# Attention turns the next heads before the probabilities, and the two feed-forward blocks are reordered at their group borders

## The reference

```python
# attention: q, k, v are (2, 8, 768, 64); proj is (64, 6)
q_bucket = sum over 6 bits of (q @ proj > 0) * 2**bit;  k_bucket likewise
scores = where(q_bucket == k_bucket, q @ k.T / 8, -1e9)
attn = exp(scores - max);  attn = attn / (sum + 1e-9);  out = attn @ v
x = out, heads side by side, (1536, 512)
# first feed-forward block, 512 -> 1536 -> 512
x = (sigmoid(x @ w_gate) * (x @ w_val)) @ w_out
# second feed-forward block, 512 -> 2048 -> 512
h = x @ w_in
g = where(h >= 1, h, where(h <= -1, 0, (h + 1)**2 / 4))
out = g @ w_out2
```

## Time and profile before

| | |
|---|---|
| median of 3 runs | 798.59 us (798.53 to 802.11) |
| profiled execution | 800.75 us, its span 799.0 us |
| granted TensorE clock, mean | 0.998 |
| PE busy | 778.3 us (97%) |
| PEld busy | 718.2 us (90%) |
| DVE busy | 564.7 us (71%) |
| ACT busy | 457.1 us (57%) |
| POOL busy | 551.4 us (69%) |

### The profile page before, as it was taken

The page is one execution under the profiler, slowest core; times in us unless marked ns, Lnnn a source line. Parts: engine busy times, 40 slices in busy tenths (PEclk is TensorE's granted clock), DMA queues, the critical chain, the costliest instruction groups (busy, mean ns, idle before and its releaser), DMA issues.

```text
span 799.0 us, 12190 instructions
## 1 busy us (share of the span) xinstructions
PE 778.3 (97%) x4403; PEld 718.2 (90%) x4403; DVE 564.7 (71%) x867; ACT 457.1 (57%) x731; POOL 551.4 (69%) x533
## 2 busy tenths in 40 slices
PE   7999999999999999999999999999999999999998
PEld 6899999998979999999899999988999988899996
DVE  5888888887888576446975655597678677666554
ACT  4888988988997424335434334454455464534543
POOL 4667767778889998877885887776657756466420
PEclk9999999999999999999999999999999999999999
DMA  7896586475100212202021221111121111101002
GB/s 146 183 191 138 134 174 139 82 153 119 54 1 27 77 58 79 77 29 79 27 80 54 80 80 53 53 54 54 37 71 53 47 32 69 65 26 53 1 1 79
DMA packets 61930, 60.08 MB, mean 75 GB/s; under 512 B 28384, under 2 KB 51632, under 8 KB 61872
## 3 DMA queue, kind: packets, MB, share of 16 engines
q1 hardware_dynamic: 61712, 59.32, 28.8%
q10 hardware_dynamic: 160, 0.00, 0.0%
HBM read 37.75 MB, written 3.15 MB: 51 GB/s over the span
## 4 chain that ended last, share of the span: by engine, by line
PE 77%; DVE 8%; ACT 6%; issue 5%; POOL 3%; DMA 0%; SPq 0%; POOLq 0%; DVEq 0%; ACTq 0%
PE ps L748 11%; PE ps L749 11%; PE ps L750 11%; PE ps L778 8%; PE ps L789 5%; PE ps L791 5%; PE ps L790 5%; PE ps L779 4%; PE ps L714 4%; ACT ph L907 2%; PE ps L731 2%; PE ps L732 2%; PE ps L702 2%; DVE probs L1200 2%; PE ps L705 2%
## 5 line engine op out<-in xcount | busy, mean ns | idle before, releaser
L748 PE MATMUL ps<-xop,wset 128*128 128x384 f32 x560 | 191.2, 341 | 5.0 <-DVE u L1276 3.9
L749 PE MATMUL ps<-xop,wset 128*128 128x384 f32 x560 | 189.5, 338 | 0.0
L750 PE MATMUL ps<-xop,wset 128*128 128x384 f32 x560 | 189.0, 338 | 0.0
L1276 DVE TENSOR_TENSOR u<-ps,u 128x384 f32<-128x384 f32 x144 | 79.5, 552 | 102.0 <-PE ps L750 101.8
L516 POOL TENSOR_TENSOR wset<-stage,wset 128x512 fp32r<-128x512 f32 x39 | 54.3, 1392 | 122.0 <-ACT wset L955 122.0
L748 PEld LDWEIGHTS ps<-xop,wset 128*128 128x128 f32 x560 | 105.4, 188 | 20.2 <-issue 8.2
L1211 DVE TENSOR_TENSOR pl<-ps,ph 128x768 fp32r<-128x768 f32 x96 | 91.4, 954 | 26.5 <-ACT ph L907 25.4
L749 PEld LDWEIGHTS ps<-xop,wset 128*128 128x128 f32 x560 | 105.5, 188 | 3.8
L491 POOL TENSOR_SCALAR probs<-probs,small 128x768 f32<-128x768 f32 x96 | 88.3, 927 | 24.9 <-DVE small L1205 22.1
L750 PEld LDWEIGHTS ps<-xop,wset 128*128 128x128 f32 x560 | 105.4, 188 | 0.0
L522 POOL TENSOR_TENSOR wset<-wsum,wset 128x1024 fp32r<-128x1024 f32 x39 | 97.1, 2489 | 0.0
(11 more groups left out here) (137 smaller groups left out, 1721.7 us busy)
## 6 DMA issues: line engine op xcount, KB each, us to landing
stage<-in_moe_w_in_dram SPq DMA_DIRECT2D x16, 512.0 KB, 3.4
stage<-in_moe_w_out_dram SPq DMA_DIRECT2D x14, 512.0 KB, 4.0
stage<-in_moe_w_gate_dram SPq DMA_DIRECT2D x12, 512.0 KB, 4.3
stage<-in_moe_w_val_dram SPq DMA_DIRECT2D x12, 512.0 KB, 3.6
ops<-qh SPq DMA_DIRECT2D x15, 384.0 KB, 5.3
ops<-kh SPq DMA_DIRECT2D x28, 192.0 KB, 5.1
qn<-in_q_dram SPq DMA_DIRECT2D x16, 192.0 KB, 4.5
kn<-in_k_dram SPq DMA_DIRECT2D x16, 192.0 KB, 5.0
```

Of the source, the lines that this page charges most:

```text
L748: pe.matmul(dst, high[:, c, :], high_x(r)[:, c, :], start=(c == 0), stop=False)
L749: pe.matmul(dst, high[:, c, :], low_x(r)[:, c, :], start=False, stop=False)
L750: last = pe.matmul(dst, low[:, c, :], high_x(r)[:, c, :], start=False, stop=(c == 1))
L1276: dve.tensor_tensor(dst, bank(n, r), other, ALU.add).then_inc(e_dve, 1)
```

## The change

Eight edits, in words:

- In attention, PE, ACT and DVE handle the next pair's Q and K ahead of the probabilities of the same step, and the list `uses` is made in that order.
- In value sets other than the second and the last of a group, DVE empties r = 6 ahead of `gate_second`.
- ACT alone copies the finished sums out of PSUM (`empty_y`); DVE's part is gone, and one semaphore stands for two.
- ACT rounds the weights of a group's second set in the group's first set, not in the set before.
- POOL's sums for that second set wait for the whole of the next x to be split (`x_low`), not for the last tile.
- In the first hinge set of a group ACT takes out the next set's r = 0 between the two halves of `hinge_part`, and DVE takes out the next set's r = 1 ahead of `add_hinge`; in the second set r = 2 and r = 3 are taken out by DVE later, between the tiles' steps.
- In the last hinge set of a group DVE's splits of x stand behind more of the tile's work.
- In the second hinge set of a group PE's eight units stand after r = 4, 5 and 6 (2, 2, 4), not after r = 2 to 6 (1, 1, 2, 2, 2).

The core of the diff:

```diff
@@ -157,10 +157,10 @@
         uses = [("Q", 0), ("K", 0)]
         for g in range(STEPS):
             uses.append(("S", g))
+            if late(g // U) <= g % U < late(g // U) + 2 and g // U < NP - 1:
+                uses.append(("QK"[g % U - late(g // U)], g // U + 1))
             if g >= LAG:
                 uses.append(("T", g - LAG))
-            if late(g // U) <= g % U < late(g // U) + 2 and g // U < NP - 1:
-                uses.append(("QK"[g % U - late(g // U)], g // U + 1))
         slot_of = {use: n % 3 for n, use in enumerate(uses)}
         before = {use: uses[n - 3] if n > 2 else None for n, use in enumerate(uses)}
         held = {n % 3: use for n, use in enumerate(uses)}
@@ -641,7 +641,7 @@
             for n in range(2, NSETS):
                 if n - 1 in FIRSTS[1:]:
 
-                    pool.wait_ge(hl_ready, 2 * pair_of(n - 2) + 2)
+                    pool.wait_ge(x_low, R * (group_of(n) + 1))
                 sums_a(n)
                 sums_b(n)
                 low_a(n)
@@ -819,7 +818,7 @@
                 if ends:
                     return (2, 2, 1, 1, 1, 1, 20)[r]
                 if n in (N1 + 1, FIRSTS[3] + 1):
-                    return (0, 0, 1, 1, 2, 2, 2)[r]
+                    return (0, 0, 0, 0, 2, 2, 4)[r]
                 return (2, 2, 1, 1, 2, 2, 2)[r]
 
             pe.wait_ge(ident_ready, 1)
@@ -841,12 +840,12 @@
             for g in range(STEPS):
                 i, u = g // U, g % U
                 scores(g)
-                if g >= LAG:
-                    turn_probs(g - LAG)
                 if u == late(i) and i < NP - 1:
                     turn("Q", i + 1)
                 if u == late(i) + 1 and i < NP - 1:
                     turn("K", i + 1)
+                if g >= LAG:
+                    turn_probs(g - LAG)
                 j, part = divmod(g - 8, HT)
                 if j >= 0:
                     weigh(j, part)
@@ -993,27 +991,33 @@
                     act.wait_ge(*emptied(n, 6 - second))
                     act.activation(hidden(pp, second), hidden(pp, second), ACT.Sigmoid).then_inc(sig_done, 1)
 
+            def hinge_relu(t):
+                act.wait_ge(clamped, t - TILES1 + 1)
+                act.activation(tile(t), tile(t), ACT.Relu, bias=minus_one).then_inc(hinge_parts, 1)
+
+            def hinge_square(t):
+                act.activation(tmp[:, :], tmp[:, :], ACT.Square, bias=half, scale=0.5).then_inc(hinge_parts, 1)
+
             def hinge_part(t):
-                m = t - TILES1
-                act.wait_ge(clamped, m + 1)
-                act.activation(tile(t), tile(t), ACT.Relu, bias=minus_one).then_inc(hinge_parts, 1)
-                act.activation(tmp[:, :], tmp[:, :], ACT.Square, bias=half, scale=0.5).then_inc(hinge_parts, 1)
+                hinge_relu(t)
+                hinge_square(t)
 
             def empty_y(g):
 
                 if g < 2:
                     act.wait_ge(tile_used, T1 * (g + 1))
-                    act.copy(x[:, g, 0:2, 0:512], ps[:, 0:2, :])
-                    act.copy(x[:, g, 0:2, 512:S], ps[:, 4, :].rearrange("p (c n) -> p c n", c=2)).then_inc(y_act, 1)
+                    act.copy(x[:, g, :, 0:512], ps[:, 0:KT, :])
+                    act.copy(x[:, g, :, 512:S], ps[:, 4:6, :].rearrange("p a (c n) -> p (a c) n", c=2)).then_inc(emptied_y, 1)
                 else:
                     act.wait_ge(tile_used, TILES1 + T2)
                     act.wait_ge(x_low, 4 * R)
-                    act.copy(osb[:, 0:HT, :], ps[:, 0:HT, :]).then_inc(y_act, 1)
+                    act.copy(osb, ps[:, 0:T, :]).then_inc(emptied_y, 1)
 
             def gate_set(n):
                 pp, g = pair_of(n), group_of(n)
                 first_product(n)
                 if n in FIRSTS:
+                    round_w(n + 1)
                     empty_y(g - 1)
                 else:
                     round_tile(2 * pp - 2)
@@ -1074,7 +1082,6 @@
                     round_x(g + 1, 6)
                     round_tile(t + 1)
                     round_x(g + 1, 5)
-                    round_w(n + 2)
 
             act.dma_start(projn[0:D, :], proj).then_inc(proj_in, 16)
             act.dma_start(projn[D:P, :], proj).then_inc(proj_in, 16)
@@ -1310,17 +1316,6 @@
                 dve.wait_ge(hinge_parts, 2 * (t - TILES1 + 1))
                 dve.tensor_tensor(tile(t), tile(t), tmp[:, :], ALU.add).then_inc(hinge_done, 1)
 
-            def empty_y(g):
-                if g < 2:
-                    dve.wait_ge(tile_used, T1 * (g + 1))
-                    dve.tensor_copy(x[:, g, 2:4, 0:512], ps[:, 2:4, :])
-                    dve.tensor_copy(x[:, g, 2:4, 512:S],
-                                    ps[:, 5, :].rearrange("p (c n) -> p c n", c=2)).then_inc(y_dve, 1)
-                else:
-                    dve.wait_ge(tile_used, TILES1 + T2)
-                    dve.wait_ge(x_low, 4 * R)
-                    dve.tensor_copy(osb[:, HT:T, :], ps[:, HT:T, :]).then_inc(y_dve, 1)
-
             def sum_ahead(n):
 
                 g = group_of(n)
@@ -1352,8 +1345,13 @@
                 empty(n, 4)
                 sum_ahead(n)
                 empty(n, 5)
-                gate_second(n)
-                empty(n, 6)
+                if n - 1 in FIRSTS or n + 1 in FIRSTS:
+
+                    gate_second(n)
+                    empty(n, 6)
+                else:
+                    empty(n, 6)
+                    gate_second(n)
                 gate_first(n)
                 if n + 1 in FIRSTS:
                     rest_tile(t)
@@ -1367,36 +1365,44 @@
             def hinge_set(n):
                 t, g = 2 * pair_of(n), group_of(n)
                 ahead = n + 1 in FIRSTS
-                empty(n, 1)
-                if n not in FIRSTS:
+                if n - 1 not in FIRSTS:
+                    empty(n, 1)
+                if n - 1 in FIRSTS:
+
+                    empty(n, 2)
                     rest_tile(t - 2)
+                    empty(n, 3)
                     add_hinge(t - 1)
-                empty(n, 2)
-                empty(n, 3)
-                if n not in FIRSTS:
-                    rest_tile(t - 1)
+                else:
+                    if n not in FIRSTS:
+                        rest_tile(t - 2)
+                        add_hinge(t - 1)
+                    empty(n, 2)
+                    empty(n, 3)
+                    if n not in FIRSTS:
+                        rest_tile(t - 1)
                 if ahead:
                     rest_x(g + 1, 0)
                 empty(n, 4)
-                if ahead:
-                    rest_x(g + 1, 1)
+                if n - 1 in FIRSTS:
+                    rest_tile(t - 1)
                 sum_ahead(n)
                 empty(n, 5)
                 clamp(t)
                 if ahead:
-                    sum_x(g + 1, 3)
+                    rest_x(g + 1, 1)
                 empty(n, 6)
                 if n in FIRSTS:
-                    empty_y(g - 1)
+                    empty(n + 1, 1)
                 add_hinge(t)
                 clamp(t + 1)
                 if ahead:
                     rest_tile(t)
+                    sum_x(g + 1, 3)
+                    add_hinge(t + 1)
                     rest_x(g + 1, 2)
-                    add_hinge(t + 1)
-                    rest_x(g + 1, 3)
                     rest_tile(t + 1)
-                    for r in MADE[4:]:
+                    for r in MADE[3:]:
                         rest_x(g + 1, r)
 
             low_turned("Q", 0)
```

38 lines of the change are left out of this document (18 added, 20 removed).

## The result

| | before | after |
|---|---|---|
| median of 5 runs each | 799.02 us (798.53 to 802.11) | 794.62 us (793.13 to 795.60) |
| profiled execution, its span | 800.75, 799.0 us | 794.62, 792.5 us |
| PE busy | 778.3 us (97%) | 776.4 us (98%) |
| POOL busy | 551.4 us | 538.3 us |

The ratio is 0.9934, its 95% interval 0.9912 to 0.9955: the kernel became 4.4 us (0.6%) faster, where 789.4, 9.2 less, had been forecast: a little under half of the forecast gain. So what an edit is worth is read from the places in the traces, and the medians are held against it.

What follows compares the result with a forecast made beforehand. PE was taken as the bound, busy 97% of the span. Terms 3.4 + 0.4 + 3.2 + 1.2 + 1.4 - 0.4 = 9.2 us, taken off the 798.59 median, gave 789.4; own range 787 to 792.5, full range 786.2 to 795.2.

Steps and rivals of the forecast that it cites:

- Value to gate: Four value sets of each of two groups: emptying r = 6 before `gate_second` gains 3.4 us (bounds 1.5 to 3.7).
- 0.3 for the new waits: Deduction in the value sets: DVE's later multiplications make P(n).3 wait 0.05 to 0.1 each, 0.3 us taken off.
- rival 5: No change: POOL's late weights (1.2 at three borders) and P(n).3 waits (0.6 in eight sets) leave 797.8; chance 0.06.
- Border to set 12: POOL starts after all splits of x, so DVE is through 3.3 us sooner; gain 0.4 us (0 to 0.6).
- Sets 24 and 25: Losses of 3.9 us (`u1`, unit's wait, half clock) go, P25.4 waits 0.7 instead; net gain 3.2 us (1.0 to 3.9).
- Rival 2's counter-argument: Against DVE being short in sets 25 and 33: the two copies alone are 1.9 us of its queue.
- The clock's 1.7: Sets 24 and 25: the half clock behind the unit's wait, 3.5 x 0.48 = 1.7 us, counted among the losses.
- Set 31: The 2.21 us split goes behind the first `clamp`, the wait before tile 38's unit goes; gain 1.2 us (0.3 to 1.2).
- set 33: Like set 25 without the clock's fall: 1.54 + 0.17 and 0.44, less a new 0.7; gain 1.4 us (0.4 to 2.1).
- Attention: Q and K ahead of probabilities only exchanges two groups around one release; 0.06 lost per pair, -0.4 us (+2.1 to -2.5).
- The step from the profile to the median: Whole forecast: profiled execution is 2.2 us above the median of 798.59; the 9.2 us taken off that median gives 789.4.
- rival 2: Borders do not pay, DVE is short in sets 25 and 33: half their gain goes, 792.7 to 795; chance 0.20.

## Why the prediction was right, and where its sizes were off

**Direction and mechanism** hold: the edits pay in the feed-forward blocks, at the places named, and attention takes a little back. Of the forecast's 9.2 us, 4.4 came. Of the 4.8 that are missing, 1.7 are in terms of the sum, 1.0 is the start of the one profile, 1.7 lie between the profiled execution of before (800.75) and its median (799.02), and 0.4 outside the span (1.75 us before, 2.15 after). The steps, in their order:

- *Value to gate, 3.4 forecast, 2.7 measured*, and 0.4 at the end of set 23. The 0.66 for each set and 0.28 in the later group are right. "0.3 for the new waits" was mis-sized: 0.98 came back at P4.3 and P6.3, nothing at P8.3 and P10.3, some 0.4 a product later in the four sets, and 0.29 at P18.0. The 0.98 is there because I took DVE's 1.33 from a set in which POOL worked beside the large multiplication alone. The run in which POOL waits shows the cause. That rival 5 asked for 0.6 in all eight sets was too dark. (The lower bound given for this term is 1.5; its own condition, 0.3 in each of eight sets, gives 3.7 - 2.4 = 1.3.)
- *Border to set 12, 0.4 forecast, 0.4 measured* (0.35 of it at P12.3), but for another reason than the one given: not the new wait of POOL, which the run that undoes it shows to be worth nothing, but, as that run's trace has it, the later rounding. POOL's late weights cost nothing at any border; the 1.2 of the bound did not appear.
- *Sets 24 and 25, 3.2 forecast, 2.25 measured.* The unit's wait is gone, and P25.4 waits in its place. "`clamp` 0.56" was mis-sized (0.91), and the 1.55 of the one in set 24 beside POOL brought a wait of 0.46 at P25.1 that no term had. Rival 2's counter-argument gave the copies too much: undoing their move costs 0.65 at P25.4 and nothing at P33.4. ACT's earlier `u1` brought 0.37 of its 0.44. The clock's 1.7 is some 1.5 by the two profiles that have the old borders and no fall.
- *Set 31, 1.2 forecast, 1.3 measured; set 33, 1.4 and 1.5*: right, with the 0.7 of the new wait in set 33 met to 0.03.
- *Attention, -0.4 forecast, -1.1 measured.* The exchange of two waits of equal length is as described. The step that failed is the look only as far as k's transposes: I followed `pl` of the first step and not that of the second, which stands behind `kl` and stops the first product of the third step, 0.17 in each pair.
- *The step from the profile to the median* is the largest single error. Taken off the median, the sum should have left out what that one execution had and the median did not. It was 2.2 above the median, and the fall of the clock, 1.7 of the 9.2, was in it. A mean granted clock of 0.998 or less, the sign of such a fall somewhere in a run, stands in only 12 of the 55 runs of the kernel before that went with the experiments. So 1.7 was counted twice over, as a gain and as a part of the 2.2. Without it the forecast would have been 799.0 (the median of before) less 7.5, that is, 791.5.
- *The start* is the other part: 1.0 of the 6.5 to 7.5 is its chance in the one profile. The fastest runs of the change, 793.13 and 793.32, stand 5.4 below the fastest of before (798.53), and the places without start and clock give 6.5 + 1.0 - 1.7 = 5.8.

The forecast's own range, 787 to 792.5, missed the median; the range to 795.2 held it by 0.6, and only because rival 2's time (792.7 to 795) was let in. Its time came true and its mechanism did not, which is luck. It took half of sets 24, 25, 31 and 33 away for want of DVE's time; measured, sets 24 and 25 fell 0.9 short, and 31 and 33 not at all. The run with r = 2 ahead of the tile wins 1.7 at P25.4 and P33.4 with the same amount of DVE's work and no new wait, so it was the order, and beside it slow instructions, and not DVE's time that was short.

On the contention of VectorE and GpSimd, the trace first. `empty`, with one input in PSUM, stays at 0.54 to 0.56 beside POOL in all rows above. The multiplications and splits, with two inputs in SBUF, go from 0.95 to 1.26 and 1.49 and from 0.55 to 1.09. The Trainium skill ("SBUF — State Buffer", Who interferes with whom) has that division, and this case agrees. `clamp` has one input, in SBUF. Where POOL stands still it takes 0.55 or 0.56, and beside POOL anything from 0.55 to 2.03. The prediction put the page's rule too widely: the page has instructions with at most one SBUF input free of contention only outside the modes that use both port pairs, and it names `tensor_scalar`, which `clamp` is, among those that can enter such a mode. So the page and the trace agree here too; that `clamp` ran in such a mode is not shown, but 0.56 for 768 columns, where a `tensor_tensor` takes 0.95, fits it. For `empty` the rule as the prediction used it holds.

## What to carry to other kernels

Put the instruction that frees a bank which TensorE will soon need ahead of the work on tiles, and place the consumer of a tile by when the tile is really done: without one changed row of a table the change gained nothing. When a forecast starts from one profiled execution, ask of each term whether the median run has it too, and take it out on both sides if not. When two groups are exchanged on an in-order engine, follow every later instruction in the pair, not only the next user of the exchanged slot.
